# Attention probabilities transposed in 32x32 blocks on VectorE, and their product with V in 32-row tiles

## What is computed

```python
# q, k, v: [4, 8, 576, 64] fp32; w_in [512, 1024], conv_w [3, 1024], w_out [1024, 512]
q_rot, k_rot = rotate(q), rotate(k)                  # rotary embedding, cos and sin tables
scores = matmul(q_rot, k_rot.T) / sqrt(64)
attn = exp(scores - max(scores)); attn /= sum(attn) + 1e-9
x = matmul(attn, v)                                  # heads laid side by side: [4, 576, 512]
h = maximum(x @ w_in, 0)
conv = sum(conv_w[k] * h shifted by k - 1 rows, k = 0, 1, 2)
y = (h * sigmoid(conv)) @ w_out
```

## Time and profile before

| | us |
|---|---|
| median of 3 runs | 621.09 |
| lowest, highest | 617.1, 622.86 |
| the profiled execution | 621.75 |
| its span, first to last instruction | 619.9 |

### The profile page before, as it was taken

One profiled execution on the slowest core, in us unless ns is written; L12 is line 12 of the kernel. 1 busy time (PEld: TensorE's weight loads), 2 busy tenths in 40 slices (PEclk: granted clock), 3 DMA queues, 4 the chain that ended last, 5 costly groups with the idle time before them and its releaser, 6 DMA issues.

```text
span 619.9 us, 11198 instructions
## 1 busy us (share of the span) xinstructions
PE 517.3 (83%) x3616; PEld 430.0 (69%) x3616; DVE 403.4 (65%) x793; ACT 323.3 (52%) x719; POOL 221.6 (36%) x233
## 2 busy tenths in 40 slices
PE   0057999889887999969987899996988799998996
PEld 0056666679886666659987666676988566667996
DVE  7876476349987666419996765626996857643531
ACT  1235577536565655425664664534665655643552
POOL 4312565626451333205550423303562143311321
PEclk9998999989999999997998999998998999998999
DMA  5878000043563000041654000013546100000011
GB/s 190 237 205 301 1 1 2 2 162 107 163 181 87 1 2 1 2 165 52 188 175 124 2 2 1 2 30 148 160 138 184 47 1 2 2 2 0 1 39 40
DMA packets 22772, 48.71 MB, mean 79 GB/s; under 512 B 3120, under 2 KB 7344, under 8 KB 21936
## 3 DMA queue, kind: packets, MB, share of 16 engines
q1 hardware_dynamic: 22704, 47.87, 25.5%
HBM read 28.98 MB, written 4.72 MB: 54 GB/s over the span
## 4 chain that ended last, share of the span: by engine, by line
PE 45%; issue 18%; DVE 17%; ACT 6%; DMA 5%; POOL 5%; SPq 2%; DVEq 0%; ACTq 0%; POOLq 0%
PE banks L393 13%; PE banks L363 7%; PE banks L330 4%; DVE conv L694 4%; DVE neg_max L648 3%; PE banks L331 3%; DVE xc L633 3%; PE banks L424 3%; PE banks L426 3%; PE banks L425 3%; PE banks L408 2%; DMA Q<-K 2%; PE banks L410 2%; PE banks L409 2%; ACT conv L535 2%
## 5 line engine op out<-in xcount | busy, mean ns | idle before, releaser
L648 DVE TENSOR_REDUCE neg_max<-banks 128x1 f32<-128x576 f32 x144 | 108.5, 756 | 71.2 <-PE banks L331 62.7
L330 PE MATMUL banks<-K,Q 128*128 128x288 f32 x256 | 85.4, 348 | 51.4 <-DMA K<-K 32.5
L810 POOL TENSOR_SCALAR P_first<-P_first,recip 128x576 f32<-128x576 f32 x68 | 50.1, 746 | 164.8 <-DVE recip L665 164.8
L814 POOL TENSOR_TENSOR u_lo<-u,u_hi 128x288 fp32r<-128x288 f32 x64 | 60.5, 946 | 108.7 <-ACT u_hi L546 108.6
L694 DVE SCALAR_TENSOR_TENSOR conv<-banks,taps,conv 128x288 f32<-128x288 f32 x128 | 65.4, 511 | 45.0 <-ACT conv L535 33.7
L408 PE MATMUL banks<-x_hi,wi_hi 128*128 128x290 f32 x256 | 81.0, 317 | 16.3 <-DVE u L702 13.9
L330 PEld LDWEIGHTS banks<-K,Q 128*128 128x128 f32 x256 | 50.4, 197 | 60.7 <-issue 32.6
L506 ACT ACTIVATE P_first<-banks,neg_max 128x576 f32<-128x576 f32 x88 | 65.1, 740 | 47.9 <-DVE neg_max L648 39.7
L363 PE MATMUL banks<-ident,P_first 128*128 128x128 f32 (+1 forms) x400 | 78.6, 288 | 12.6 <-DVE P_first L771 3.1
L424 PE MATMUL banks<-u_hi,wo_hi 128*128 128x288 f32 x256 | 77.2, 302 | 5.1 <-ACT y_sb L552 5.1
L410 PE MATMUL banks<-x_hi,wi_lo 128*128 128x290 f32 x256 | 79.4, 310 | 0.0
(11 more groups left out here) (66 smaller groups left out, 1052.8 us busy)
## 6 DMA issues: line engine op xcount, KB each, us to landing
xc<-qk_dram SPq DMA_DIRECT2D x28, 288.0 KB, 2.8
xs<-qk_swapped_dram SPq DMA_DIRECT2D x28, 288.0 KB, 3.9
V<-v_rows_dram SPq DMA_DIRECT2D x4, 1280.0 KB, 6.2
KL<-Q SPq DMA_DIRECT2D x32, 144.0 KB, 3.6
Q<-K SPq DMA_DIRECT2D x32, 144.0 KB, 3.7
K<-K SPq DMA_DIRECT2D x32, 144.0 KB, 2.7
y_dram<-y_sb SPq DMA_DIRECT2D x8, 576.0 KB, 3.3
wi_raw<-w_in_dram SPq DMA_DIRECT2D x1, 2048.0 KB, 8.1
```

Source lines behind the costliest of these rows:

```text
L330: nc.tensor.matmul(out, Q[:, h, qc], K[:, h, cols], start=True, stop=False)
L648: nc.vector.tensor_reduce(out=neg_max[:, c:c + 1], in_=banks[:, 2 * (t % 2):2 * (t % 2) + 2, 0:HALF], axis=AX.XY, op=ALU.max, negate=True) ...
L810: nc.gpsimd.tensor_scalar(p, p, recip[:, c:c + 1], 1.0, ALU.mult, ALU.mult).then_inc(normed, 1)
```

## The change

- TensorE's transposes, their PSUM copies on ScalarE and VectorE, and the identity are gone. VectorE transposes each normalised tile once, in 32x32 blocks, from SBUF to SBUF (`turn`, one instruction of 128x576 float32 for a tile), four tiles behind its maximum (`BEHIND`).
- `times_v` goes over 18 blocks of 32 keys, four quadrants of 32 partitions (each holds another 32 queries of every 128) and two heads: 144 matmuls to a pair, 32 rows by 64 columns of the array, with 128 or 160 moving columns, into four PSUM banks. They are issued in five chunks (4, 4, 4, 3, 3 key blocks) behind five tiles' scores, 5 to 9 tiles after the pair's last tile; the last pair's stand at the end, behind all of `early_hidden`.
- V is repeated in all four quadrants and loaded pair by pair into two buffers (1152 KB each; two at the start).
- `x_high` and `x_low` are three instructions each, for the order in which the queries lie.
- `add_eps` moves from VectorE to GpSimd; `times_sin` of all batches but the first moves from GpSimd to VectorE. The weight splits are spread over tiles 8 to 32.

```diff
+    BEHIND = 4
+    CHUNKS = [(0, 4), (4, 8), (8, 12), (12, 15), (15, NB)]        # NB = S // 32
-        T0, PV0 = 4, 6
+        T0, PV0 = 4, 4
+        WEIGHTS_AT = [8, 11, 14, 17, 20, 24, 28, 32]
+        def values_at(pair, chunk):
+            return min(TILES * (pair + 1) + BEHIND + 1 + chunk, N_SCORES - 1)
...
+            def load_v(b, pair):
+                sp.dma_start(V[:, pair % 2, :, :, :], v_rows[b, pair, :, :, :, :]).then_inc(v_in[pair % 2], 16)
...
                     if starting and j == 6:
-                        sp.dma_start(V[:, :, :, :], v_rows[0, :, :, :, :]).then_inc(v_in, 16)
+                        load_v(0, 0)
+                        load_v(0, 1)
...
+            def times_v(b, pair, chunk):
+                if chunk == 0:
+                    pe.wait_ge(turned_done, b * N_SCORES + TILES * (pair + 1))
+                    pe.wait_ge(v_in[pair % 2], b * 32 + 16 * (pair // 2 + 1))
+                    if pair > 0:
                         pe.wait_ge(x_split, b * PAIRS + pair)
+                for k in range(*CHUNKS[chunk]):
+                    for a in range(4):
+                        rows = slice(32 * a, 32 * a + 32)
+                        for n in range(2):
+                            tiles, cols = turned_of(pair, n, a)
+                            last = nc.tensor.matmul(banks[n * D:(n + 1) * D, PV0 + a, cols], V[rows, pair % 2, n, k, :],
+                                                    turned[rows, tiles, 32 * k:32 * k + 32],
+                                                    start=(k == 0), stop=(k == NB - 1))
+                if chunk == len(CHUNKS) - 1:
+                    last.then_inc(pv_done, 1)
...
             def attention(b):                                       # tensor
+                for t in range(AHEAD, N_SCORES):
+                    score(b, *tile_at(t))
+                    for pair in range(PAIRS - 1):
+                        for chunk in range(len(CHUNKS)):
+                            if t == values_at(pair, chunk):
+                                times_v(b, pair, chunk)
+                for n in range(4):
                     early_hidden(b, n)
+                for chunk in range(len(CHUNKS)):
+                    times_v(b, PAIRS - 1, chunk)
...
+            def times_sin(g, j):                                    # vector
+                _, w = rope_buffers(j, False)
+                nc.vector.tensor_tensor(w, w, sin_t[:, :], ALU.mult).then_inc(sin_done, 1)
...
+            def turn(b, t):                                         # vector
+                pair, i = tile_at(t)
+                dve.wait_ge(*tile_normed(b, pair, i))
+                if pair > 0 and i == FULL + 1:
+                    dve.wait_ge(pv_done, b * PAIRS + pair)
+                nc.vector.transpose(turned[:, turned_slot(pair, i), :], p_tile(pair, i)).then_inc(turned_done, 1)
...
+                turn(b, 0)                                          # attention(b), vector
+                turn(b, 1)
+                for t in range(AHEAD, N_SCORES + BEHIND):
+                    if t < N_SCORES:
+                        max_tile(b, *tile_at(t))
+                    turn(b, t - BEHIND)
...
+                        if t == values_in(pair) + 2:                # values_in: the tile of the last chunk
+                            x_low(b, pair)
```

More of the change, by code:

```diff
@@ L145, in p_tile, with turned_slot, turned_of, tail_cols @@
         def p_tile(pair, i):
[L147 to L151, removed]
+            return P[:, tiles_before(pair, i) % AHEAD, :]
+        def turned_slot(pair, i):
+            if pair % 2 == 0 or i > FULL:
+                return i
+            return 2 * FULL + 1 if i == FULL else 2 * FULL + 2 + i
+        def turned_of(pair, n, a):
+            has_tail = a // 2 == n
+            main = turned_slot(pair, n * (FULL + 1))
+            first = (turned_slot(pair, FULL) < main) and has_tail
+            s, c = (main - 1, 0) if first else (main, 32)
+            count = FULL + has_tail
+            return slice(s, s + count), slice(c, c + 32 * count)
+        def tail_cols(pair, n):
+            c = turned_of(pair, n, 2 * n)[1].start
+            return slice(0, 32) if c == 0 else slice(32 * (FULL + 1), 32 * (FULL + 2))
         def tile_normed(b, pair, i):
@@ L174, in stat, with tile_at @@
             return TILES * (pair % 2) + i
[L176 to L192, removed]
         FIRST_TILES = [(0, i) for i in range(FULL + 2)]
+        def tile_at(t):
+            return t // TILES, t % TILES
         def tiles_before(pair, i):
             return pair * TILES + i
[L198 to L215, removed]
         def weight_chunk(h):
@@ L344, in score @@
                 score_tile(b, tiles_before(pair, i), pair, i)
[L346 to L365, removed]
@@ L367, in transpose_tail @@
-            def transpose_tail(b, h):
-                n = unit_of(None)
-                pair, r = h // 2, other_rows(h)
-                bank_free(b, h, n)
-                pe.wait_ge(*tile_normed(b, pair, FULL))
-                alone(pe)
-                for kt in range(KT):
-                    m = 128 if kt < FULL else TAIL
-                    last = nc.tensor.transpose(banks[0:m, T0 + n % 2, kt * TAIL:(kt + 1) * TAIL],
-                                               p_tile(pair, FULL)[r, kt * 128:kt * 128 + m], ident[r, r])
-                last.then_inc(transposed, 1)
@@ L554, in attention @@
             def attention(b, first):
-                late = FIRST_TILES[-1]
-                for h in range(H):
-                    for n, (kt, tile) in enumerate(slots(h)):
-                        if late:
-                            exp_tile(b, *late)
-                        late = tile
-                        if n % 2 == 0:
-                            copy_pt(b, h, kt)
-                        if first and kt == FULL:
-                            weights_high(h)
-                    if h >= 2 and h % 2 == 0:
-                        x_high(b, h // 2 - 1)
+                for t in range(AHEAD - 1, N_SCORES):
+                    exp_tile(b, *tile_at(t))
+                    for pair in range(PAIRS - 1):
+                        if t == values_in(pair):
+                            x_high(b, pair)
+                    if first and t in WEIGHTS_AT:
+                        weights_high(WEIGHTS_AT.index(t))
                 load_table(ACT.Sigmoid)
@@ L846, in gated_mlp @@
                         u_low(b, n - 2)
-                    if not last and n % 2 == 1 and n // 2 < H:
-                        times_sin(b + 1, n // 2)
                 if not last:
@@ L869 @@
     B, H, S, D = q.shape
-    half, full = D // 2, S // 128
+    half = D // 2
     dm, ff = moe_w_in.shape
```

197 lines of the change are left out of this document (71 added, 126 removed).

## The result

| | before | after |
|---|---|---|
| median, us | 619.1 | 601.37 |
| lowest, highest, us | 617.0, 622.86 (4 runs) | 601.04, 603.58 (4 runs) |
| ratio | | 0.9715, 95% interval 0.9654 to 0.9776 |
| span of the profiled execution, us | 619.9 | 599.2 |
| granted TensorE clock, mean of the span | 0.973 | 0.906 |

The change makes the kernel 2.9% faster; the forecast was 609 us, with a range of 580 to 690. The total is near, but it is not made of the terms that I summed. One term put at zero was worth -13 us, one at 28 us was worth about 6, and the start and a place that I left out took back about 11.

A forecast was written before the change was run, and what follows sets the result against it. Attention was taken as bound by TensorE's issue order, with VectorE the next limit. From the profiled 621.75 us, -17 (attention, four batches) + 4 (start) + 0 (sine) = -13 gave 609 us, range 580 to 690.

The forecast's parts named there:

- one at 28 us: Attention: low TensorE clock at product starts, +2 us a pair and +1 us a batch on early hidden tiles.
- Product with V: Attention on TensorE: all eight array tiles run at once, 4.86 us a pair as before; upper end 19.4 us.
- the two rivals: Product in attention: records start too slowly (688 us at 40 ns; 0.24), or row quadrants run serially (813 us; 0.11 with other serial costs).
- The transpose: VectorE in attention: one 576-column tile transpose takes 0.75 us, with ends of 0.68 and 1.37.
- The half-rate rival: VectorE in attention: a transpose takes 1.37 us, +9.9 us a batch, total 649 us; chance 0.06.
- The sum of one batch: Attention from tile 6's score to the last `x_low`: 73.8 us against 78.0, -4.2 a batch, -17 in four.
- each pair's first chunks run at 1.2 GHz: TensorE in attention: low clock for about 4 us, costing +2 us a pair, because transposes leave its slots emptier.
- the stretches ahead and behind are left alone: Outside tile 6's score to the last `x_low`: nothing changes but the separately counted V-load and sine terms.
- The start: First loads: 1.05 MB more V ahead of the weights delays the chain by +4 us (3.5 to 6).
- The sine product: MLP stage: moving it from GpSimd to VectorE counts 0, ends -10 and +12 us over three batches.
- the likeliest case: Whole kernel: eight tiles at once and low clock at each chunk row's start; own range 595 to 618 us, chance 0.35.
- the clock holds: Attention: TensorE keeps full clock, -11.2 us a batch, total 581 us; chance 0.12.

The follow-up runs named there:

- experiment 1: Changed kernel with the row quadrant as the outer loop of a product chunk, same matmuls: 817.5 us in the profiled run.
- experiment 2: Changed kernel with 64 moving columns instead of 128 or 160 in all product matmuls but the first key block's: 588.9 us, ratio 0.9474.
- experiment 5: Changed kernel with two extra unread 224-column matmuls per half score tile in slots without a product chunk: 595.4 us, ratio 0.959.
- experiment 7: Changed kernel with V of the second pair loaded behind the weights at the start: 598.5 us, ratio 0.9649.
- experiment 4: Sine product of batches 1 to 3 put back on GpSimd in the changed kernel: 614.5 us; moved to VectorE alone in the kernel before: 606.8 us.

## Why the prediction was right, step by step

- **Product with V**: right, and for the reason given. Eight tiles at once, 4.8 us a pair; experiments 1 and 2 put the two rivals aside.
- **The transpose**: 0.765 us for 0.75. The half-rate rival (1.37) is out.
- **The sum of one batch**: it gave 73.8 us for 78.0. The same stretch of after in batch 2, from the score of tile 6 at 333.68 to 406.71, is 73.0. But two of its terms were off against each other. The step "each pair's first chunks run at 1.2 GHz", 7 us a batch with the hidden tiles, is about 2 by experiment 5, because only one pair's first chunk of the three is reached by the low level; the other 5 stand in small costs that I had at nothing. A slot with a four-block chunk takes 2.02 us (349.17 - 347.14), for 0.53 + 0.15 + 1.08 = 1.76; over 14 slots that is up to 3.6. The last product stands still for 0.98 us. What the low clock does cost is, in part, the shared tile's eight matmuls, for which VectorE waits 1.04 us (timeline of after, VectorE):

```profile
346.42 0.76 DVE L603 TENSOR_REDUCE neg_max<-banks 128x1 f32<-128x576 f32 x1 [1.04 <-PE banks L335]
```
- **What lay outside that stretch**: the failed step is "the stretches ahead and behind are left alone". With `BEHIND` = 4, two transposes stand ahead of tile 6's maximum, here in the timeline of after:

```profile
333.49 1.43 DVE L628 STREAM_TRANSPOSE turned<-P 128x576 f32<-128x576 f32 x2
334.84 0.72 DVE L603 TENSOR_REDUCE neg_max<-banks 128x1 f32<-128x576 f32 x1
```

  Tile 5's and tile 6's maxima are 2.83 us apart, 1.48 before: +1.35 us a batch, 5 us in all, that no term held.
- **The start**: I had 0 for the first batch (-4.2 + 4). Its attention ended 6 us later than before. The weights were 2.4 us late, less than the 4, but the first batch's own gain did not come: tiles are held by the late weights and by GpSimd's splits, so VectorE's and TensorE's shorter work is not on the path there. That is seen in the chain; experiment 7 shows only the 2.9 us for the load, and the rest is not separated. The clock may have a part in it. In before, TensorE's matmuls reach their full-speed length at 47.1 us and lose it from 57.4 to 64.2; in after they stay at 442 ns until 67.0, here from 50 to 66.5:

```profile
L337 PE MATMUL banks<-K,Q x12: 442/442/609, 50.1 to 66.2; 128*128 128x288 f32 x12
```

  The profile has no record of the grant before 47.1 us in before and 67.0 in after, and its 1.00 there can't be read as full clock.
- **The sine product**: the mis-sized term, 0 for -13 us. Its range, -10 to +12, did not hold it. I had the numbers (1.509 against 0.812) but set TensorE's 40 of 45.5 us behind it as the next limit, and left out two things. TensorE's limit lay at the 41.8 us of the last batch's MLP and not at 45.5, with VectorE's 42.8 us of work above it; and the rotary step has a tail. Behind the last tap the next tile 6 came 19.5, 19.5 and 18.0 us later with the sine on GpSimd, against 17.6, 17.6 and 17.5 (experiment 4).
- **The sum of it**: forecast -17 + 4 + 0. Measured: attention with the start and the tiles ahead of it, and all that is not the sine, -5; the sine -13. The forecast was 8 us too high: 5 us in the change, and 2.7 because it started from the profiled 621.75 us and the median of before is 619.1. It came so near only because the errors went both ways, which is luck. Of the likeliest case the eight tiles came true and the low clock at each pair did not; its own range, 595 to 618 us, holds the time.
- **The rivals**: "the clock holds" (581 us) didn't come, since the grant fell in every batch (13.6 us at 0.50 ahead of pair 0's chunks, 6.8 around the start of pair 1's in batches 2 and 3, 3.4 in the hidden tiles); and the 28 us that this would have been worth by my terms shrank to 6 in experiment 5.

## What to carry to other kernels

Small matmuls are cheap when neighbours in the order go to different row quadrants and column halves, and dear when they don't: write the quadrant as an inner loop. Before a term is put at zero because another engine is "nearly full", look for a stage with the same work on that engine and less beside it (here the last batch's MLP), which shows how far the time can fall, and count what two-tensor work on GpSimd costs VectorE's two-tensor work beside it. When work goes from TensorE to VectorE, the stretches that VectorE then paces can lose TensorE's clock (0.51 here); some spare matmuls in them were worth 1%.

## What the runs showed of the hardware that I had not expected

- Records of 32x64 tiles begin 7 ns apart, and sustain 11 ns with 64 columns and 17 ns with 128 and 160, where the largest matmuls of the kernel before came every 121.5 ns.
- With the quadrants one after the other, the next one begins 0.61 us after this one although a tile's eight records take 0.86 to 1.08 us: TensorE runs ahead across the seam.
- The last product of each looping batch stops at the same place, between its 238 and 50 records, for 0.98 us in batch 2 of after. The profile's DMA view lists packets of a queue that it calls instruction; between 400.7 and 402.0 there is one, of 16 KB, which has landed 1.4 us before the matmul that ends the stop at 403.40 (packets, MB, share of 16 engines):

```profile
q8 instruction: 1, 0.02, 5.7%
```

  Nine runs have such stops, 35 in all, and in each a packet of this queue lands 1.2 to 1.5 us before the matmuls go on. The place moves with the number of instructions ahead of it (behind 262 records in experiment 5), the stop is longer where records are shorter (1.9 to 2.2 us in experiment 2), and with the quadrants apart, 36 ns to a record, there is none. So these stops are waits for instructions to be fetched, as far as traces can tell; no run was made to test it.
- From the last `x_low` to the first tap it takes 1.7 us in the first and last batch of after and 4.9 and 4.7 in the two where the loop goes round (2.5 against 5.7 and 5.4 in before).
- A busy TensorE does not always have its clock: with the quadrants apart the grant was 0.50 for 122.9 us in which TensorE was busy for 115.9 (experiment 1).
- Idle slots move the grant, and the loss is small where the low level falls on work that VectorE paces anyway: in the three later batches 62 us of attention at the low level became 18, and that gave some 6 us.
